# A spatial gating block on one Trainium2 core: the bias is added by VectorE instead of by a two-row product, and the transposes behind the scan are placed differently

## The reference

```python
# 1: a recurrence over 768 steps, each head with a 48x48 state
for t in range(S):
    cur = np.einsum('bhd,bhe->bhde', u[None] * kt, vt)
    y[:, :, t] = np.einsum('bhd,bhde->bhe', rt, state + cur)
    state = wt[:, :, :, None] * state + np.einsum('bhd,bhe->bhde', kt, vt)
# 2: x is y as (2, 768, 384); a normalised feed-forward with 1536 hidden features
ch = np.maximum(xn @ w_ch1, 0.0) @ w_ch2
x = x + ch
# 3: a gated block, d_ff = 1024, with a 768x768 product over time
h = np.maximum(x @ w_in, 0.0)
u, v = (h[..., :d_ff // 2], h[..., d_ff // 2:])
v_n = (v - mu) / np.sqrt(var + 1e-06)
v_s = np.einsum('ts,bsd->btd', w_spatial, v_n) + b_spatial[None, :, None]
gated = u * v_s
return (gated @ w_out).astype(np.float32)
```

## Time and profile before

| | us |
|---|---|
| median of the three runs | 429.12 |
| the three runs | 428.51, 429.12, 432.5 |
| the profiled execution's own time (it is the run of 432.5) | 432.5 |
| its span, first to last instruction | 430.7 |
| outside the span | 1.8 |
| TensorE busy | 403.1 (94%) |
| VectorE busy | 222.3 (52%) |
| ScalarE busy | 147.5 (34%) |
| GpSimd busy | 127.2 (30%) |
| mean granted TensorE clock | 0.968 |

### The profile page before, as it was taken

How to read it: one execution, slowest core, us unless ns; L and a number is a source line. 1 busy time by engine, 2 the same in 40 slices (tenths; PEclk the granted TensorE clock), 3 DMA queues, 4 the chain that set the end, 5 groups by cost and what they waited for, 6 DMA issues and landing times.

```text
span 430.7 us, 12369 instructions
## 1 busy us (share of the span) xinstructions
PE 403.1 (94%) x5260; PEld 375.0 (87%) x5260; DVE 222.3 (52%) x492; ACT 147.5 (34%) x328; POOL 127.2 (30%) x149
## 2 busy tenths in 40 slices
PE   3687789999999999999999899999999999999997
PEld 2576677999999999999999799999988988989897
DVE  2788777656667666667543444133246934312120
ACT  3334544253442323232424422322227712211111
POOL 3577666636442423323221421001015400000000
PEclk9997885899999999999999999999999999999999
DMA  7914541503201020110000200000061100010102
GB/s 201 330 38 129 169 136 47 154 20 112 76 22 53 20 58 15 31 67 2 3 2 2 75 2 0 0 2 2 0 221 33 42 0 0 7 50 21 37 20 91
DMA packets 26555, 24.60 MB, mean 57 GB/s; under 512 B 1666, under 2 KB 23426, under 8 KB 26500
## 3 DMA queue, kind: packets, MB, share of 16 engines
q1 hardware_dynamic: 26500, 23.80, 17.9%
HBM read 21.44 MB, written 2.36 MB: 55 GB/s over the span
## 4 chain that ended last, share of the span: by engine, by line
PE 89%; DVE 4%; issue 3%; POOL 2%; DMA 1%; ACT 1%; SPq 0%; DVEq 0%; POOLq 0%; ACTq 0%
PE odd_bank L1214 11%; PE odd_bank L1216 9%; PE odd_bank L1215 9%; PE low_bank L1133 7%; PE low_bank L1214 6%; PE low_bank L1216 6%; PE low_bank L1215 6%; PE high_bank L1214 4%; PE high_bank L1215 4%; PE high_bank L1216 4%; PE bank L1181 3%; PE bank L1216 3%; PE bank L1215 3%; PE bank L1214 3%; PE bank L1177 2%
## 5 line engine op out<-in xcount | busy, mean ns | idle before, releaser
L566 POOL TENSOR_TENSOR kin<-kin,wtot 128x256 f32<-128x256 f32 x60 | 48.4, 814 | 67.3 <-PE low_bank L1133 62.6
L1133 PEld LDWEIGHTS low_bank<-rin,kin 64*64 64x64 f32 x1728 | 31.9, 144 | 19.7 <-issue 8.0
L1133 PE MATMUL low_bank<-rin,kin 64*64 64x32 f32 x1728 | 36.5, 229 | 13.3 <-DVE rin L831 5.7
L831 DVE TENSOR_TENSOR rin<-rin,wtot 128x256 f32<-128x256 f32 x60 | 36.4, 611 | 14.2 <-PE low_bank L1133 12.1
L961 DVE SCALAR_TENSOR_TENSOR h10l<-odd_bank,h10h 128x384 fp32r<-128x384 f32 x24 | 13.4, 558 | 44.7 <-ACT h10h L705 44.7
L583 POOL TENSOR_TENSOR vrstd<-vmv,half 128x1 f32<-128x1 f32 x12 | 7.7, 643 | 70.9 <-DVE vmv L1046 70.9
L564 POOL TENSOR_TENSOR kin<-kin,win 128x256 f32<-128x256 f32 x12 | 12.9, 1076 | 51.6 <-PE low_bank L1133 47.5
L873 DVE COPY_PREDICATED near<-msk,low_bank 128x256 f32<-128x256 int32 x54 | 27.0, 552 | 0.0
L1214 PE MATMUL odd_bank<-xnT0h,ffw 128*128 128x384 f32 x66 | 25.0, 379 | 0.0
L705 ACT ACTIVATE h11h<-odd_bank 128x384 fp32r<-128x384 f32 x16 | 7.9, 492 | 47.7 <-PE odd_bank L1216 47.7
L1215 PE MATMUL odd_bank<-xnT0l,ffw 128*128 128x384 f32 x66 | 22.7, 344 | 0.0
(11 more groups left out here) (252 smaller groups left out, 1156.7 us busy)
## 6 DMA issues: line engine op xcount, KB each, us to landing
kin<-in_kT SPq DMA_DIRECT2D x12, 256.0 KB, 3.3
rin<-in_rT SPq DMA_DIRECT2D x12, 256.0 KB, 4.3
win<-in_wT SPq DMA_DIRECT2D x12, 256.0 KB, 5.2
early_stage<-in_w SPq DMA_DIRECT2D x8, 384.0 KB, 5.6
vin<-in_v SPq DMA_DIRECT2D x12, 192.0 KB, 3.2
out<-ob SPq DMA_DIRECT2D x12, 192.0 KB, 1.9
stage<-in_w SPq DMA_DIRECT2D x4, 384.0 KB, 5.7
stage<-in_w_in SPq DMA_DIRECT2D x4, 384.0 KB, 3.2
```

Of the source, the lines that this page charges most:

```text
L566: last = gp.tensor_tensor(k, k, wr[:, :, :, None].to_broadcast([P, NPR, m, c]), ALU.mult)
L831: last = ve.tensor_tensor(r, r, wl[:, :, :, None].to_broadcast([P, NPR, m, c]), ALU.mult)
L1133: mm = te.matmul(dst[s0:s0 + Q, NPR * e + a, :], kin[i % 4][lo:hi, a, s0:s0 + Q], r[:, :, 1, :], start=True, stop=True)
```

## The change

The bias is now a tile `bias` of 128 rows of 768, all rows alike; the host gives it so, and one load of 384 KB brings it in. The bias product and the five operations of `bias_split` are gone; the first of the 18 products starts the sum. VectorE takes an SP sum from PSUM by adding the bias (`gf`), which sets the new semaphore `spatial_taken`, does the remainder of the block before (`gated_lo(m - 1)`), and then multiplies `gf` by u in place. TensorE waits for `spatial_taken` in place of `gated_ready`. In `ff_steps` the X2T turns of group 0 stand at m = 0, 2, 3 instead of 0, 1, 2, and those of group 3 behind the second, third and fourth U of group 2 instead of behind the first, second and third.

```diff
-        bias_hl = sb("bias_hl", [2, S], F32R)
-        ones_r = sb("ones_r", [2, P], F32R)
+        bias = sb("bias", [P, S])
...
-                for g, at_x2t, at_v, at_u in ((0, 0, 5, 6), (1, 7, 10, 11), (2, 12, 15, None)):
-                    if at_x2t <= m < at_x2t + TG:
-                        yield "X2T", g, m - at_x2t
+                for g, at_x2t, at_v, at_u in ((0, (0, 2, 3), 5, 6), (1, (7, 8, 9), 10, 11), (2, (12, 13, 14), 15, None)):
+                    if m in at_x2t:
+                        yield "X2T", g, at_x2t.index(m)
...
             for d in range(ND):
                 yield "U", NG - 2, d
-                if d < TG:
-                    yield "X2T", NG - 1, d
+                if d:
+                    yield "X2T", NG - 1, d - 1
...
-            for row in range(2):
-                sp.dma_start(bias[row:row + 1, :], b_sp).then_inc(bias_step, 16)
+            sp.dma_start(bias[:, :], b_sp).then_inc(bias_loaded, 16)
...
-            def bias_split(part):
...
-                    elif n - N_BESIDE - 1 < 4:
-                        bias_split(n - N_BESIDE - 1)
...
+            def gated_lo(m):
+
+                j, a = m // ND, m % ND
+                dve.wait_ge(gated_hi_ready, m + 1)
+                ve.tensor_tensor(gT[j % 2][1][:, a, :], gf[m % 2][:, :], gT[j % 2][0][:, a, :].bitcast(F32),
+                                 ALU.subtract).then_inc(gated_lo_ready, 1)
+
+            dve.wait_ge(bias_loaded, 16)
...
-                ve.tensor_tensor(gf[m % 2][:, :], b_f1[m % 2][:, 0:GT], uT[:, a, j * GT:(j + 1) * GT],
+                ve.tensor_tensor(gf[m % 2][:, :], b_f1[m % 2][:, 0:GT], bias[:, j % 2 * GT:(j % 2 + 1) * GT],
+                                 ALU.add).then_inc(spatial_taken, 1)
+                if m:
+                    gated_lo(m - 1)
+                dve.wait_ge(spatial_taken, m + 1)
+                ve.tensor_tensor(gf[m % 2][:, :], gf[m % 2][:, :], uT[:, a, j * GT:(j + 1) * GT],
                                  ALU.mult).then_inc(gated_ready, 1)
-                dve.wait_ge(gated_hi_ready, m + 1)
-                ve.tensor_tensor(gT[j % 2][1][:, a, :], gf[m % 2][:, :], gT[j % 2][0][:, a, :].bitcast(F32),
-                                 ALU.subtract).then_inc(gated_lo_ready, 1)
                 if j < 2 and m < CH:
                     split_vn(CH + m)
+            gated_lo(ND * NG - 1)
...
-            te.wait_ge(bias_step, 37)
...
-                        te.wait_ge(gated_ready, m - 1)
+                        te.wait_ge(spatial_taken, m - 1)
                     o = b_f1[m % 2][:, 0:GT]
-                    te.matmul(o, ones_r[:, :], bias_hl[:, tg * GT:(tg + 1) * GT], start=True, stop=False)
                     for c in range(CH):
...
-                                           False, c == CH - 1)
+                                           c == 0, c == CH - 1)
```

More of the change, by code:

```diff
@@ L120, in rwkv_moe_kernel @@
         vn = place("vn", [P, NT, DH])
-        bias_at = at[0]
         uT = place("uT", [P, ND, B * S])
@@ L130, in rwkv_moe_kernel @@
         ff_end = at[0]
-        bias = nc.alloc_sbuf_tensor_at("bias", [2, S], F32, offset=bias_at)
-        bias_hi = nc.alloc_sbuf_tensor_at("bias_hi", [2, S], F32R, offset=bias_at + 4 * S)
-        ones = nc.alloc_sbuf_tensor_at("ones", [2, P], F32, offset=bias_at + 8 * S)
         at[0] = ff_tokens
@@ L282, in rwkv_moe_kernel @@
         vn_lo_ready = sem("vn_lo_ready")
-        bias_step = sem("bias_step")
+        bias_loaded = sem("bias_loaded")
         spatial_done = sem("spatial_done")
+        spatial_taken = sem("spatial_taken")
         gated_ready = sem("gated_ready")
@@ L1066, in _ @@
                 m = ND * j + a
-                sl = slice(a * P, (a + 1) * P)
                 if m == 0:
@@ L1390 @@
         "w_sp": by_row_tile(np.ascontiguousarray(moe2_w_spatial.T)),
-        "b_sp": np.ascontiguousarray(moe2_b_spatial.reshape(1, S)),
+        "b_sp": np.ascontiguousarray(np.broadcast_to(moe2_b_spatial, (P, S))),
         "w_out": by_row_tile(moe2_w_out),
```

## The result

| | before | after |
|---|---|---|
| median us (lowest to highest) | 428.81 (428.21 to 432.5, 4 runs) | 417.65 (417.25 to 417.92, 4 runs) |
| profiled execution, own time | 432.5 | 417.79 |
| its span | 430.7 | 416.0 |

The changed kernel is faster: the ratio is 0.9717, with a 95% interval of 0.9684 to 0.975, 11.2 us from median to median. The forecast was 416.6 us in a range of 414.5 to 421.0.

The account below looks back on a forecast made before the run. Behind the scan, TensorE's own list plus two waits was taken to bound the kernel. Gains of 9.4 + 2.2 + 0.9 = 12.5 us from the median 429.12 gave 416.6 us, range 414.5 to 421.0.

Parts of the forecast that it names:

- Bias products: TensorE's output part: 16 two-row products removed, each costing 0.57 to 0.59 us and not 0.17; gain 9.4 us.
- The edge: TensorE, last product of one spatial sum to second of the next: 0.92 us before, two steps of 0.35 without bias product.
- Turns: Moved X2T turns no longer wait for VectorE: 2.16 us gained in group 0, 0.93 us in group 3.
- The spare times: Claimed margins: 1.4 us before V(3,0) needs its remainder, 3.2 us before TensorE needs the last gated block's.
- VectorE's chain: Output steps that split v_n: add through ScalarE's roundings to the split, at most 3.5 us against a sum every 3.12.
- The slip: VectorE's next add falling behind by at most 0.4 us a step; cost put at nothing, bounds 0 to 2.3 us.
- The load: Bias of 384 KB ahead of two w_in chunks, 3.2 us to landing; cost taken as nothing, 3.2 without cover.
- The slot alone: Rival: late starts belong to the edge, so only 2.8 us of bias products go, 5.9 in all: 423.2 us; 5%.
- VectorE's pace: Rival: VectorE sets the pace in steps that split v_n, giving 2.3 us back: 418.9 us; 8%.
- the passed-on wait: Rival: turns gain nothing because the next turn or V waits as long, leaving 9.4 us: 419.7 us; 5%.
- the last of these: Rival: a new wait for spatial_taken drops the clock in the output part, slower than before, 435.3 us; 2%.
- the waits of 2.0 and 0.7 us: TensorE's only two waits from 236 us on in the profile before, both ahead of a turn, with the clock at 1.00.

Follow-up runs that it names:

- the second comparison: The changed kernel run once more beside the kernel before on the same chip: 416.84 us against 430.47, ratio 0.9679.
- the three comparisons: The changed kernel against the kernel before: first run, repetition, and with an unused tile added to restore the scan's addresses; ratios 0.9717, 0.9679 and 0.967.
- a sixth: Repetition of the kernel before with only the bias moved to VectorE, turns in the old order: 421.1 us against 429.87, ratio 0.9776.

## Why the prediction was right

- **What bounds.** TensorE's list behind the scan set the time, in every kernel: each change of the list came out of the tail to within 0.1 us of its term (with the 64-row product 0.24).
- **Bias products, 9.4 us.** 9.43 measured alone. The edge without it is 0.35 us as expected, and sums are 3.12 apart. The rule that a product over 32 rows takes as long as one over 128 ("TensorE: Matmul & The Clock Gate" of the Trainium skill, "Why this matters for your kernels") would have priced it at 2.8 us. It is no price for such a product between others of 128 rows: the two runs with widened rows put the difference of 6.66 us on the change of the row count. The page "TensorEngine Tiling (Array Packing)" of the Trainium skill says, under "Key Properties", that a change of the tiling mode drains the engine; the two runs agree with it, though no row shows the drain itself.
- **Turns, 3.1 us.** 3.12 measured alone, no wait passed on. The spare times hold too: VectorE had the remainder of the first turn of group 3 at 323.65 + 0.55 = 324.2, 1.3 us ahead of V at 325.54 (1.4 forecast), and the last gated block's at 403.3, 3.4 us ahead of the output sum that needs it, at 406.69 (3.2 forecast). On VectorE, and the start of that sum on TensorE:

```profile
323.65 0.55 DVE L916 TENSOR_TENSOR xnT0l<-odd_bank,xnT0h 128x384 fp32r<-128x384 f32 x1
...
402.73 0.56 DVE L1044 TENSOR_TENSOR gT1l<-gf,gT1h 128x384 fp32r<-128x384 f32 x1 [0.58 <-ACT gT1h L763]
```

```profile
406.69 0.33 PE L1201 MATMUL bank<-ffw,gT1h 128*128 128x384 f32 x1
```

- **VectorE's chain.** The bound of 3.5 us a step was 3.21, since operations start up to 0.1 us before the one ahead has ended (344.97 - 344.49 = 0.48 for an add of 0.56). The slip was there, 0.08 us a step, and cost nothing, the value taken.
- **The load.** It landed in 2.9 us (KB, median us from issue to landing), ahead of the two chunks of w_in, and nothing waited:

```profile
bias<-in_b_sp SPq DMA_DIRECT2D x1, 384.0 KB, 2.9
```

- **The total.** 416.6 was forecast and 417.65 measured; the second comparison gave 416.84. The difference is in the scan, for which the range was given 4 us. The forecast took the same gain for the whole time as for the tail. A gain of 12.45 of 430 us is a ratio of 0.971; the three comparisons have 0.9717, 0.9679 and 0.967, so one alone is off by up to 1.7 us. The gain of the tail, 12.44 of 12.5, is the test of the mechanism; that the total came within 1.1 us is in part luck.
- **Rivals.** The slot alone (423.2) fell with the edge, VectorE's pace (418.9) and the passed-on wait (419.7) with the empty view of waits, and the clock stayed at 1.00 behind the scan in the profile after. Against the last of these I had held that the waits of 2.0 and 0.7 us left the clock alone; in one of six profiles the first did not. The rival needed such a wait in the output part, and there was none.

## What to carry to other kernels

Price an instruction by the distance of starts on both sides of it, not by its length or its size: a product of another row count in a dense list cost two late starts beside its slot here, and it can be cheaper to fill it up with zero rows than to leave it narrow. Moving work to an engine with slack is free only if its longest chain through the other engines fits the period, and the order that looks better pipelined (the old remainder first) may feed the other engine later. Where a stage that varies by more than the change stands ahead of it, compare the stretch behind it, which repeated to hundredths here unless the clock fell in it, and look at the granted clock first.

## What was not expected of the hardware

The late starts with 64 rows are as long as with 2 (0.27, 0.37 and 0.28 us between starts in place of 0.17), the weight load starts with its product there and not 0.17 us ahead, and 16 bias products over 128 rows, 126 of them zeros, are 6.66 us cheaper than those over 2. A wait of TensorE of 2.0 us left the clock alone in five profiles and was followed by about 3 us at the lower level in a sixth, which is a repetition of one of the five. And the scan, with the same list in 13 profiles, ended anywhere between 231.78 and 238.66 us, all of it made ahead of about 80 us.
